# Order of the six down tiles of a unit: two blocks of three instead of three blocks, in the order of TensorE and of VectorE

## The reference, cut to what matters

```
x = attention(q, k, v)                    # 4 batches, 8 heads, 576 tokens of 64
P = sinkhorn(exp(x @ w_gate), 8 steps)    # 2304 tokens, 8 experts
out1 = sum over e of P[:, e] * (relu(x @ w1[e]) @ w2[e])     # 512 -> 1024 -> 512
out  = elu(out1 @ w_in) @ w_out                              # 512 -> 2048 -> 512
```

## Time and profile before

| | us |
|---|---|
| three runs | 2036.92, 2040.68, 2040.81 |
| median | 2040.68 |
| the profiled execution | 2047.78 |
| its span in the profile | 2046.0 |
| PE busy in it | 2019.0 |
| DVE busy | 1433.8 |
| ACT busy | 901.9 |
| POOL busy | 1162.7 |

### The profile page before, as it was taken

One profiled execution on the slowest core, in us unless ns is written; L12 is line 12 of the kernel. 1 busy time (PEld: TensorE's weight loads), 2 busy tenths in 40 slices (PEclk: granted clock), 3 DMA queues, 4 the chain that ended last, 5 costly groups with the idle time before them and its releaser, 6 DMA issues. The chain is left out here.

```text
span 2046.0 us, 29802 instructions
## 1 busy us (share of the span) xinstructions
PE 2019.0 (99%) x10611; PEld 1829.4 (89%) x10611; DVE 1433.8 (70%) x2462; ACT 901.9 (44%) x1659; POOL 1162.7 (57%) x1519
## 2 busy tenths in 40 slices
PE   7999999999999999999999999999999999999999
PEld 6888999999999999999999998999999999998998
DVE  5775877766667676666666778776666666778876
ACT  5763333333333333333333577443333333377775
POOL 3455656455556575555555567666545555657663
PEclk9998999999999999999999999999999999999999
DMA  7631122222112222211222222322212221222221
GB/s 140 128 64 62 62 62 83 62 71 75 62 62 81 64 62 62 83 62 62 73 72 63 64 71 64 102 62 76 70 62 73 72 62 65 80 63 63 93 72 53
DMA packets 159299, 147.69 MB, mean 72 GB/s; under 512 B 64432, under 2 KB 126128, under 8 KB 159152
## 3 DMA queue, kind: packets, MB, share of 16 engines
q1 hardware_dynamic: 159152, 145.79, 24.5%
HBM read 141.05 MB, written 4.72 MB: 71 GB/s over the span
## 5 line engine op out<-in xcount | busy, mean ns | idle before, releaser
L508 POOL TENSOR_TENSOR w_lo<-w_raw,w_hi 128x256 fp32r<-128x256 f32 x480 | 354.2, 767 | 747.0 <-ACT w_hi L857 747.0
L1126 DVE SCALAR_TENSOR_TENSOR acc<-psum,prob_eps,acc 128x512 f32<-128x512 f32 x516 | 387.1, 751 | 273.8 <-PE psum L732 273.1
L732 PE MATMUL psum<-w_hi,h_lo 128*128 128x512 f32 x1440 | 563.8, 392 | 0.0
L730 PE MATMUL psum<-w_hi,h_hi 128*128 128x512 f32 x1440 | 562.1, 390 | 0.6 <-issue 0.6
L731 PE MATMUL psum<-w_lo,h_hi 128*128 128x512 f32 x1440 | 561.1, 390 | 0.0
L671 PE MATMUL psum<-x_hi_a,w_hi 128*128 128x384 f32 x1296 | 438.1, 338 | 4.5 <-DVE c L1093 3.7
L674 PE MATMUL psum<-x_hi_a,w_lo 128*128 128x384 f32 x1296 | 438.7, 338 | 0.0
L673 PE MATMUL psum<-x_lo_a,w_hi 128*128 128x384 f32 x1296 | 437.0, 337 | 0.0
L501 POOL TENSOR_TENSOR w_lo<-s_tmp,w_hi 128x256 fp32r<-128x256 f32 x480 | 356.1, 773 | 0.0
L732 PEld LDWEIGHTS psum<-w_hi,h_lo 128*128 128x128 f32 x1440 | 270.5, 188 | 56.2
L730 PEld LDWEIGHTS psum<-w_hi,h_hi 128*128 128x128 f32 x1440 | 270.3, 188 | 42.8 <-issue 0.9
(11 more groups left out here) (118 smaller groups left out, 2752.2 us busy)
## 6 DMA issues: line engine op xcount, KB each, us to landing
w_raw<-in_moe_w_dram SPq DMA_DIRECT2D x192, 512.0 KB, 3.6
w_raw<-in_moe_w_in_dram SPq DMA_DIRECT2D x24, 512.0 KB, 3.4
w_raw<-in_moe_w_out_dram SPq DMA_DIRECT2D x24, 512.0 KB, 3.7
v_l<-in_v_dram SPq DMA_DIRECT2D x24, 128.0 KB, 3.5
out_dram<-acc SPq DMA_DIRECT2D x2, 1536.0 KB, 6.7
raw_l_q<-in_q_dram SPq DMA_DIRECT2D x8, 288.0 KB, 4.9
raw_l_k<-in_k_dram SPq DMA_DIRECT2D x8, 288.0 KB, 5.6
raw_s_q<-in_q_dram SPq DMA_DIRECT2D x16, 144.0 KB
```

The lines of the kernel that those rows point to most:

```text
L508: pool.tensor_tensor(w2_lo[n % 2][piece], w2_raw[piece], w2_hi[n % 2][piece].bitcast(f32), ALU.subtract).then_inc(w2_lo_s, 1)
L730: pe.matmul(dst, h_hi[:, i, kk, js], w2_hi[s][:, i, :], start=(i == 0), stop=False)
L732: mm = pe.matmul(dst, h_lo[:, i, kk, js], w2_hi[s][:, i, :], start=False, stop=(i == 1))
L1126: ins = dve.scalar_tensor_tensor(a, y, 1.0 if bare else gate_of(n, j), a, ALU.mult, ALU.add)
```

## The change

TensorE does p4(n) after tile 5 of u, right before p3(n), where it had been between tile 3 and tile 4; so tiles 3, 4 and 5 stand together. VectorE makes C21(n) at the end of the turn, after tile 5 is evicted (and after `join`, in the turns that have one), where it had been after tile 3; the steps that read it (the sum and the low part of H21) move into the next turn, after C12(u) and before the low part of H22. The sum of H22 moves from before tile 4's eviction to after it. ScalarE, GpSimd and SyncE are as before.

```diff
@@ TensorE, the turn of unit u
                     p2(n)
                     p7(n)
                 down(u, HT)
-                if more:
-                    p4(n)
                 if u < SINKHORN_STEPS:
                     sum_columns(u)
                 down(u, HT + 1)
                 down(u, HT + 2)
                 if more:
+                    p4(n)
                     p3(n)
@@ VectorE, the turn of unit u
                 if u >= 0:
                     make_c12(u)
                     if is_elu(u):
+                        elu_sum(u, E21, c21[:, :], c21[:, :])
+                        elu_lo(u, H21, c21[:, :])
                         elu_lo(u, H22, c22[:, :])
                     else:
+                        relu_lo(u, H21, c21[:, :])
                         relu_lo(u, H22, c22[:, :])
                         relu_lo(u, H12, c12[u % 2][:, :])
...
                 if more:
                     if is_elu(n):
                         elu_lo(n, H11, elu[E11][:, :])
-                    make_c21(n)
                     for x in x_splits(n)[1:]:
                         split_x(*x)
-                    if is_elu(n):
-                        elu_sum(n, E22, c22[:, :], c22[:, :])
                 if u >= 0:
                     evict(u, 4)
-                if more:
-                    if is_elu(n):
-                        elu_sum(n, E21, c21[:, :], c21[:, :])
-                    else:
-                        relu_lo(n, H21, c21[:, :])
+                if more and is_elu(n):
+                    elu_sum(n, E22, c22[:, :], c22[:, :])
                 if u >= 0:
                     evict(u, 5)
                 if U_BARE < u <= U_BARE + GT:
                     join(u - U_BARE - 1)
-                if more and is_elu(n):
-                    elu_lo(n, H21, c21[:, :])
+                if more:
+                    make_c21(n)
```

## The result

The changed kernel takes 2057.19 us (median of six runs, 2051.23 to 2058.34), the kernel before in the same session 2039.91 (six runs, 2036.92 to 2042.99). The ratio is 1.0072, interval 1.0058 to 1.0086, so it is slower by 0.72% or about 14.7 us. (The two medians differ by 17.3 us: the six runs of the changed kernel fall into two near 2051.5, with a mean granted clock of 0.998, and four from 2056.7 to 2058.3, with 0.993 to 0.995.) The forecast was slower by 21.7 us, 2062, range 2048 to 2078: right in direction and range, but the measured change is only some two thirds of the forecast one.

A forecast was written before the change was run, and what follows sets the result against it. TensorE, busy 2019.0 of 2046.0 us, was taken to bound the kernel. The terms -1 - 4.8 + 17.5 + 2.5 + 5.1 + 2.4 = +21.7 us, on the median 2040.7, gave 2062, range 2048 to 2078.

The forecast's parts named there:

- a block less in expert units: TensorE's extra step from tile to product and back, up to 0.01 us over 119 units, saved: -1 us.
- waits for C12 gone: TensorE's four waits for VectorE's C12 go, since C12 now precedes the low parts: -4.8 us.
- tile 0 in 23 ELU units: Tile 0 waits for the low part of H21: +17.5 us in units with x splits, +2.5 in the last phase.
- last unit, the chain: Unit 119, with no p1, p6, p5 behind p3: tile 0 waits for the low part of H21, +2.4 us.
- Expert units: The 96 expert units: C21 and the low part of H21 come in time, cover 1.3 us or more; price 0.
- The chain: ELU units: C21's end to H21's low part, 3.42 us; ready 4.17 after p3 starts, as is tile 0; 0.15 a unit.
- ScalarE's lag: ScalarE's turn 1.35 us later against TensorE, so the second `turn_back` waits 0.85 in six ELU units: +5.1 us.
- the x splits: ELU units with x splits: VectorE makes C21 late, delaying tile 0; 8.75 us, twice 17.5.
- 0.4 late: Turn of unit 67: U3 on VectorE starts at 1229.2 in place of 1228.74, behind ScalarE's later x part.
- the lower bound (9): Low end for all tile 0 waits: 9 us if long steps fall elsewhere and the weight load hides the 0.15.
- the two estimates at m = 3 and 6: GpSimd's sums beside the chain, a quarter of 1.4 us: 0.35 at m = 3, 0.3 at m = 6.
- The last rival: Much slower: GpSimd's queue lies beside the chain in every ELU unit, 28 us more, 2090; chance 0.10.

The follow-up runs named there:

- experiment 1: Against the kernel before: the new order only in turns whose next unit is an expert unit, the old one before ELU units; ratio 0.9997.
- Experiment 6: Changed kernel with the minus one of H21 over 8 columns in place of 384; 1860.9 us from tile 0 of unit 1, 7.2 less than the changed kernel.
- experiment 3: Changed kernel with ScalarE's first `y_copy` before the last weight split; 1864.3 us from tile 0 of unit 1, 3.9 less than the changed kernel.
- experiment 5: Changed kernel with GpSimd's sums of x ahead of the low parts of the weight sums; 1865.9 us from tile 0 of unit 1.
- experiments 2: Changed kernel with p4 and C21 one tile earlier in ELU turns; ratio 1.0017 to the kernel before, 1857.4 us from tile 0 of unit 1.
- experiment 9: As experiments 2, with the sum of H21 ahead of C12 in VectorE's order; ratio 1.0028, 1858.7 us from tile 0 of unit 1.

## Why the prediction was right, and where it was off

Point by point, from tile 0 of unit 1 to the end, in us:

| term | predicted | measured |
|---|---|---|
| a block less in expert units | -1 | -1.7 (experiment 1) |
| waits for C12 gone | -4.8 | -5.1 |
| tile 0 in 23 ELU units | +20.0 | +12.4 |
| second `turn_back`, six times | +5.1 | +4.4 |
| last unit, the chain | +2.4 | +2.4 |
| last unit, behind the pause | 0 | +1.5 |
| sum | +21.7 | +13.9 (+14.1 from the traces) |

The measured terms are differences of starts of matmuls against the usual step, added over the units; for tile 0 they are 10.6 us of pauses and 23 times 0.08 us for the step behind. Part of the 0.2 us between the two sums is in the next few steps behind a pause, each a little longer than usual.

- **The gain** was right in kind; the step out of a block and the one into it cost 0.02 us together.
- **Expert units** cost nothing, as said; experiment 1 shows it.
- **The chain** was right: 3.42 forecast, 3.41 measured, and 0.19 us a clean unit for the 0.15 taken. No row had shown the 0.05 for the signal; the runs show 0.10 from the end of the low part of H21 to tile 0, and 0.08 in the step behind it. Experiment 6 ties the 0.19 to the chain.
- **ScalarE's lag** was right, 0.74 for 0.85, and experiment 3 ties it to that lag.
- **The failed term** is that of the x splits, +20.0 for 12.4. The forecast made C21 late at m = 4, 5 and 6 and left the chain as it was, but for a quarter of a long step at m = 3 and 6. C21 was on time in all of them. "0.4 late" was wrong: ScalarE's x part came 1.2 later against tile 3, not 1.35, and VectorE's took 1.00 us, not the average of 1.24, so U3 began as far behind p7 as before; C21 was 0.3 early, not 0.2 late. And "the long ones add: the low part of H11 1.4, the sum of H22 1.2" took lengths from the kernel before for steps whose neighbour on GpSimd, as the forecast itself said of GpSimd's queue, had moved. What was long instead were steps of the chain. So m = 4 cost 1.1 in place of 2.95 and m = 5 0.7 in place of 1.55, both through the chain, and m = 3 and m = 6 the clean 0.19 in place of 0.5 and 0.65. m = 0 and m = 7, which have no such steps but a second x split, cost 1.3 (1.2 forecast) and 1.2 (1.6), through a late C21. Of the two conditions of the lower bound (9) one came true, "the long steps fall elsewhere once GpSimd's queue has moved". 20.0 less their 7.6 is 12.4, as measured, but that is luck: the 1.4 that GpSimd cost the chain in each of two phases happens to make up for smaller terms that did not come, among them the two estimates at m = 3 and 6.
- **The missing term** is the clock behind the last pause.
- **The rule weighed**, from the Trainium skill (SBUF — State Buffer, Who interferes with whom): a GpSimd instruction that reads SBUF and a VectorE instruction with two SBUF inputs exclude each other. In experiment 5 the sum of H22 began at 1232.88, GpSimd's instruction ran from 1231.84 for 2.24 us to 1234.08, and the sum ended at 1234.49, 0.41 behind it; that agrees. The low part of H11, which began 0.03 before GpSimd's, had its usual 0.56. Who began first decided. In the changed kernel the sum of H21 at m = 5 ended at 1246.38, 0.40 behind the end of that GpSimd instruction (1245.98). The last rival, built on this, came true at m = 4 and m = 5 alone. In clean units GpSimd is idle beside the chain's steps on VectorE: in the turn of unit 66 it ends at 1212.05, and the sum of H21 starts at 1213.05.

What stays open: that the waits at m = 0 and 7 come from a late C21 is read from the traces; how they divide between the x split and the two evictions that now stand ahead of C21 was not tried.

## What to carry to other kernels

Before a result is moved behind work that "had to be done anyway", follow it through every engine to its next reader and compare that length with the room that is left: here 4.17 us against 4.17. A result used by a simple step and by a six-step one needs its order chosen for each kind of unit; the change was good for 96 units and bad for 24. When a queue moves, the lengths of steps that are long only because of their neighbour must not be carried over from the old trace, and when one step is moved forward in a queue, price what it now holds up.

## What was not expected of the hardware

After a pause of TensorE the granted clock fell to its lower level for some 3.4 us in the changed kernel and in experiments 2, 3 and 6 (the last unit's tile 0 starts 3.4, 2.6, 3.4 and 3.1 us behind p3's last matmul) and once in the middle of the units, in experiment 9, where p5 started 2.2 us behind p6 at m = 4; it cost about 1.5 us each time at the end (13.1 to 13.2 against 11.6). It did not in experiment 5 with the same 3.4 us pause, nor in the kernel before, where p5 started 2.0 us behind p6. What decided between the two is open. So a pause of two or three microseconds can cost more than itself, and need not.
